# An attention, gating and expert kernel: value rows loaded straight from the input, and softmax denominators taken from a column of ones

## The reference

```python
for c in range(S // 32):
    k_full = concat(mem_k, k[:, :, max(0, 32*c - 16):min(S, 32*c + 40)])
    v_full = concat(mem_v, v[...same rows...])
    scores = q_c @ k_full.T / sqrt(64)
    a = exp(scores - scores.max(-1))
    a = a / (a.sum(-1) + 1e-9)
    out_c = a @ v_full
```

## Time and profile before

| | us |
|---|---|
| median of three runs | 2741.96 (2741.23 to 2748.13) |
| the profiled execution | 2741.23 |
| its span in the trace | 2739.5 |
| PE busy | 2662.7, 97% |
| DVE, ACT, POOL busy | 1388.3, 770.8, 516.0 |

### The profile page before, as it was taken

The page is one execution under the profiler, slowest core; times in us unless marked ns, Lnnn a source line. Parts: engine busy times, 40 slices in busy tenths (PEclk is TensorE's granted clock), DMA queues, the critical chain, the costliest instruction groups (busy, mean ns, idle before and its releaser), DMA issues.

```text
span 2739.5 us, 36851 instructions
## 1 busy us (share of the span) xinstructions
PE 2662.7 (97%) x15264; PEld 2196.0 (80%) x15264; DVE 1388.3 (51%) x2039; ACT 770.8 (28%) x1301; POOL 516.0 (19%) x440
## 2 busy tenths in 40 slices
PE   7779999999999999999999999999999999999999
PEld 6667878878777888888888888888888888888887
DVE  2454554454558454454564554544546544545544
ACT  3444332232333333333332221222222212222211
POOL 0036520020254545545430000000001000000000
PEclk8899999999999999999999999999999999999999
DMA  9946553433355565555545334333333443343342
GB/s 217 194 112 242 218 190 145 162 141 139 146 173 173 196 207 173 203 200 177 209 153 199 128 131 165 127 140 156 127 149 147 158 159 137 127 168 128 131 165 89
DMA packets 138454, 445.23 MB, mean 163 GB/s; under 512 B 34608, under 2 KB 94000, under 8 KB 106800
## 3 DMA queue, kind: packets, MB, share of 16 engines
q1 hardware_dynamic: 138288, 442.88, 45.9%
HBM read 315.97 MB, written 133.43 MB: 164 GB/s over the span
## 4 chain that ended last, share of the span: by engine, by line
PE 92%; DVE 3%; issue 2%; POOL 1%; ACT 1%; DMA 0%; DVEq 0%; ACTq 0%; POOLq 0%
PE bank L729 44%; PE bank L804 44%; PE bank L651 2%; PE bank L666 1%; PE bank L691 1%; PE bank L678 1%; POOL X L572 1%; DVE tmp L1232 1%; PE bank L701 0%; DVE Y L1265 0%; DVE Y L1323 0%; ACT X L987 0%; DVE hid L1328 0%; DVE hid L1384 0%; PE bank L706 0%
## 5 line engine op out<-in xcount | busy, mean ns | idle before, releaser
L729 PE MATMUL bank<-X,W 128*128 128x512 f32 x5550 | 1397.1, 390 | 14.8 <-ACT tmp L1035 4.9
L729 PEld LDWEIGHTS bank<-X,W 128*128 128x128 f32 x5550 | 1040.1, 188 | 240.4 <-issue 20.6
L804 PE MATMUL bank<-W,hid 128*128 128x512 f32 x4608 | 1153.7, 389 | 2.4 <-DVE Y L1262 2.4
L804 PEld LDWEIGHTS bank<-W,hid 128*128 128x128 f32 x4608 | 864.5, 188 | 182.3 <-DVE Y L1262 2.8
L1262 DVE SCALAR_TENSOR_TENSOR Y<-bank,gate,Y 128x512 f32<-128x512 f32 x720 | 539.7, 750 | 567.8 <-PE bank L804 560.4
L572 POOL TENSOR_TENSOR X<-Y,X 128x1024 fp32r<-128x1024 f32 x30 | 77.9, 2599 | 1025.1 <-ACT X L987 1025.0
L1093 ACT ACTIVATE hid<-tmp 128x512 fp32r<-128x512 f32 x192 | 121.3, 632 | 354.7 <-DVE tmp L1229 274.6
L804 PE MATMUL bank<-hid,W 128*128 128x512 f32 x864 | 219.5, 390 | 1.2 <-issue 1.2
L1031 ACT ACTIVATE tmp<-bank 128x512 f32<-128x512 f32 x132 | 78.8, 597 | 487.1 <-PE bank L729 487.1
L1384 DVE SCALAR_TENSOR_TENSOR hid<-bank,hid 128x512 fp32r<-128x512 f32 x192 | 132.7, 691 | 162.9 <-ACT hid L1093 162.8
L804 PEld LDWEIGHTS bank<-hid,W 128*128 128x128 f32 x864 | 162.4, 188 | 35.5 <-issue 1.6
(11 more groups left out here) (85 smaller groups left out, 1062.5 us busy)
## 6 DMA issues: line engine op xcount, KB each, us to landing
W<-w_kept SPq DMA_DIRECT2D x88, 1792.0 KB, 8.7
w_kept<-W SPq DMA_DIRECT2D x44, 1792.0 KB, 6.7
W<-w_kept SPq DMA_DIRECT2D x76, 1024.0 KB, 4.9
w_kept<-W SPq DMA_DIRECT2D x38, 1024.0 KB, 4.9
raw<-in_moe_w_dram SPq DMA_DIRECT2D x64, 512.0 KB, 6.4
Kr<-in_k_dram SPq DMA_DIRECT2D x12, 512.0 KB, 6.1
Qr<-in_q_dram SPq DMA_DIRECT2D x12, 512.0 KB, 7.8
Vw<-v_rows SPq DMA_DIRECT2D x48, 128.0 KB
```

The source lines that it names most:

```text
L729: last = nc.tensor.matmul(into[:, :], W1[:, c % 2, ws, w_slot, kc, :], X[:, pos, xs, kc, :], start=(start and kc == 0 and n == 0), stop=(k ...
L804: last = nc.tensor.matmul(into[:, :], lhsT, rhs, start=(j == 0 and n == 0), stop=(j == 1 and n == 2))
```

## The change

`v_rows`, `vm_rows` and the copies inside DRAM go. `load_v` reads `v` and `mem_v` directly, one chunk and one of its three kinds of rows at a time: 24 DMAs for a quad instead of six, each with rows of 64 elements (256 bytes) instead of 256 (1 KB). `Vw` has six slots instead of four, one for each quad of a batch, and each head gets a 65th column that POOL sets to one at the start. With it `weigh_v` yields the denominator as a 65th output column, DVE reads it from PSUM, and `denominators`, `esum` and `clear` go. The rows outside the sequence are never loaded; their values are cleared once at the start, and so are their ones. Two weight loads (`load_up(0)`, `load_up(1)`) move ahead of `load_v(5)`.

```diff
-            Vw = sb("Vw", [P, VS, 4, HP, HD], F32, first)
+            Vw = sb("Vw", [P, G, 4, HP, HD + 1], F32, first)
...
-            def rows_v(b, lo, hi, done):
-                for f in range(2):
-                    for s0, s1, at in ((lo, hi, lo), *([(0, LEFT, -LEFT)] if lo == 0 else []),
-                                       *([(S - RIGHT, S, S)] if hi == S else [])):
-                        sp.dma_start(v_rows[b, f, LEFT + at:LEFT + at + s1 - s0, :].rearrange("s (h d) -> s h d", h=HP),
-                                     v[b, f::2, s0:s1, :].rearrange("h s d -> s h d")).then_inc(done, 16)
...
             def load_v(r):
-                b, g, slot = r // G, r % G, r % VS
-                if r >= VS:
-                    sp.wait_ge(a_o, r - VS + 1)
...
-                for f in range(2):
-                    into = Vw[64 * f:64 * f + 64, slot].rearrange("p c h d -> p c (h d)")
-                    of = v_rows[b, f, g * QUAD:g * QUAD + QUAD, :].rearrange("(c s) n -> s c n", s=CHUNK)
-                    sp.dma_start(into[0:CHUNK], of).then_inc(s_v[slot], 16)
...
+                b, g = r // G, r % G
+                if b > 0:
+                    sp.wait_ge(a_o, r - G + 1)
+                for f in range(2):
+                    for c in range(4):
+                        start = g * QUAD + c * CHUNK - LEFT
+                        s0, s1 = max(start, 0), min(start + WIN, S)
+                        at = 64 * f + s0 - start
+                        sp.dma_start(Vw[at:64 * f + CHUNK, g, c, :, 0:HD],
+                                     v[b, f::2, s0:start + CHUNK, :].rearrange("h s d -> s h d")).then_inc(s_v[g], 16)
+                        at = 64 * f + BLK
+                        sp.dma_start(Vw[at:at + s1 - start - CHUNK, g, c, :, 0:HD],
+                                     v[b, f::2, start + CHUNK:s1, :].rearrange("h s d -> s h d")).then_inc(s_v[g], 16)
+                        at = 64 * f + CHUNK
+                        sp.dma_start(Vw[at:at + MEM, g, c, :, 0:HD],
+                                     mem_v[b, f::2].rearrange("h m d -> m h d")).then_inc(s_v[g], 16)
...
+            sp.wait_ge(s_zero, 8)
             load_v(0)
...
+            nc.gpsimd.memset(Vw[:, :, :, :, HD:HD + 1], 1.0).then_inc(s_zero, 1)
+            nc.gpsimd.memset(Vw[:, G - 1, 3, :, 0:HD], 0.0).then_inc(s_zero, 1)
+            pool.wait_ge(s_zero, 4)
+            for f in range(2):
+                nc.gpsimd.memset(Vw[64 * f:64 * f + LEFT, 0, 0], 0.0).then_inc(s_zero, 1)
+                ones = Vw[64 * f + 32:64 * f + 64, G - 1, 3, :, HD:HD + 1]
+                nc.gpsimd.affine_select(out=ones, in_=ones, compare_op=ALU.is_ge, fill=0.0, base=32 - RIGHT - 1,
+                                        pattern=[[0, HP], [0, 1]], channel_multiplier=-1).then_inc(s_zero, 1)
...
-            def clear(r):
-                pool.wait_ge(a_exp, r + 1)
...
             def weigh_v(r):
...
-                            last = nc.tensor.matmul(b_o[f][32 * c:32 * c + 32, hp * HD:(hp + 1) * HD],
+                            last = nc.tensor.matmul(b_o[f][32 * c:32 * c + 32, hp * (HD + 1):(hp + 1) * (HD + 1)],
                                                     PT[rows, hp, c * CHUNK:(c + 1) * CHUNK],
-                                                    Vw[rows, r % VS, c, hp, :], start=True, stop=True)
+                                                    Vw[rows, r % G, c, hp, :], start=True, stop=True)
...
-            def denominators(r):
-                dve.wait_ge(a_exp, r + 1)
...
             def quotients(r):
                 dve.wait_ge(a_o, r + 1)
+                for f in range(2):
+                    nc.vector.tensor_scalar(rsum[:, f, :], b_o[f][:, 0:HP * (HD + 1)].rearrange(
+                        "p (j n) -> p j n", j=HP)[:, :, HD], EPS, None, ALU.add).then_inc(a_den, 1)
+                dve.wait_ge(a_den, 2 * r + 2)
+                nc.vector.reciprocal(rsum[:, :, :], rsum[:, :, :]).then_inc(a_rs, 1)
                 dve.wait_ge(a_rs, r + 1)
```

More of the change, by code:

```diff
@@ L63, in build @@
     UNITS = 4 * TH + 1
-    VS = 4
     BLK = CHUNK + MEM
@@ L113, in build @@
             nmax = sb("nmax", [P, 2, HP], F32, first)
-            esum = sb("esum", [P, HP, 2], F32, first)
-            rsum = sb("rsum", [P, HP, 2], F32, first)
+            rsum = sb("rsum", [P, 2, HP], F32, first)
             KT1 = sb("KT1", [P, HP, KCOLS], F32, first)
@@ L131, in build @@
         w1_kept = nc.dram_tensor("w1_kept", [2 * V1 + V2, P, 4 * NP * P], F32).ap()
-        v_rows = nc.dram_tensor("v_rows", [B, 2, LEFT + S + 2 * RIGHT, HP * HD], F32).ap()
-        vm_rows = nc.dram_tensor("vm_rows", [B, 2, MEM, HP * HD], F32).ap()
         w2_kept = nc.dram_tensor("w2_kept", [V1 + V2, P, 4 * D], F32).ap()
@@ L148, in build @@
         s_q = [sem(f"s_q{i}") for i in range(TH)]
-        s_v = [sem(f"s_v{i}") for i in range(VS)]
-        s_vr = [sem(f"s_vr{i}") for i in range(TH + B - 1)]
+        s_v = [sem(f"s_v{i}") for i in range(G)]
         s_zero = sem("s_zero")
@@ L160, in build @@
         a_exp = sem("a_exp")
-        a_pad = sem("a_pad")
-        a_sum = sem("a_sum")
         a_pt = sem("a_pt")
@@ L293, in first_use @@
             return BUILDS.index(w) if w in BUILDS else None
[L297 to L301, removed]
         MK, KU, QU = range(3)
@@ L354, in load_mem, with load_v @@
                 sp.dma_start(Mk[:, :, :], mem_k[b].rearrange("h m d -> m h d")).then_inc(s_mk, 16)
-            def rows_v(b, lo, hi, done):
+            def load_v(r):
+                b, g = r // G, r % G
+                if b > 0:
+                    sp.wait_ge(a_o, r - G + 1)
                 for f in range(2):
-                    for s0, s1, at in ((lo, hi, lo), *([(0, LEFT, -LEFT)] if lo == 0 else []),
-                                       *([(S - RIGHT, S, S)] if hi == S else [])):
-                        sp.dma_start(v_rows[b, f, LEFT + at:LEFT + at + s1 - s0, :].rearrange("s (h d) -> s h d", h=HP),
-                                     v[b, f::2, s0:s1, :].rearrange("h s d -> s h d")).then_inc(done, 16)
-                    if lo == 0:
-                        sp.dma_start(vm_rows[b, f].rearrange("m (h d) -> m h d", h=HP),
-                                     mem_v[b, f::2].rearrange("h m d -> m h d")).then_inc(done, 16)
@@ L452, in _ @@
             load_q(0, 0)
-            rows_third(0)
             load_k(0, 1)
-            rows_third(1)
+            sp.wait_ge(s_zero, 8)
             load_v(0)
@@ L459, in _ @@
             load_v(1)
-            rows_third(2)
             load_q(0, 2)
@@ L466, in _ @@
             load_v(3)
-            rows_batch(1)
             load_k(1, 1)
@@ L470, in _ @@
             load_q(1, 1)
+            load_up(0)
+            load_up(1)
             load_v(5)
             load_k(1, 2)
-            load_up(0)
-            load_up(1)
             sp.wait_ge(s_wgz, 1)
@@ L487, in _ @@
                 if b < B and g == 3:
-                    rows_batch(b)
                     load_k(b, 1)
@@ L533, in _ @@
                                     base=0, pattern=[[-1, P]], channel_multiplier=1).then_inc(s_zero, 1)
+            nc.gpsimd.memset(Vw[:, :, :, :, HD:HD + 1], 1.0).then_inc(s_zero, 1)
[6 more added lines that the diff above has]
+                                        pattern=[[0, HP], [0, 1]], channel_multiplier=-1).then_inc(s_zero, 1)
+            pool.wait_ge(s_zero, 8)
             nc.gpsimd.memset(wg[:, :, :], 0.0).then_inc(s_wgz, 1)
@@ L536, in _ @@
             for c in range(KC):
-                pool.wait_ge(s_zero, 3 + c)
+                pool.wait_ge(s_zero, 9 + c)
                 done = nc.gpsimd.affine_select(out=fold[:, :], in_=fold[:, :], compare_op=ALU.not_equal, fill=1.0,
@@ L573, in operand_lo @@
                                         ALU.subtract).then_inc(x_lo, 1)
-            def clear(r):
-                pool.wait_ge(a_exp, r + 1)
[L578 to L591, removed]
             up_sums(0)
             up_lo(0)
[L594 to L599, removed]
+            for i in range(len(X_POOL)):
                 operand_lo(0, 0, i)
@@ L672, in transpose_p @@
                 pe.wait_ge(a_exp, r + 1)
-                if edge(r):
-                    pe.wait_ge(a_pad, edges_to(r))
                 if r > 0:
@@ L682, in weigh_v @@
                 pe.wait_ge(a_ptc, r + 1)
-                pe.wait_ge(s_v[r % VS], 6 * 16 * (r // VS + 1))
+                pe.wait_ge(s_v[r % G], 24 * 16 * (r // G + 1))
                 if r > 0:
@@ L822, in gates_fold @@
                 if t == 0:
-                    pe.wait_ge(s_zero, 3 + KC)
+                    pe.wait_ge(s_zero, 9 + KC)
                 for m in range(SUB):
@@ L1170, in quotients @@
                 for f in range(2):
-                    nc.vector.tensor_tensor(On[:, :, f, :],
-                                            b_o[f][:, 0:HP * HD].rearrange("p (j n) -> p j n", j=HP),
```

(5 more changed lines are left out.)

## The result

The changed kernel takes 2819.06 us (median of four runs, 2817.98 to 2820.31) against 2741.8, a ratio of 1.0276 with a 95% interval of 1.0259 to 1.0294. It is slower by 77 us. The forecast was 2812, within a range of 2788 to 2866.

A forecast was written before the change was run, and what follows sets the result against it. The attention stage, bound by transfers, would become bound by SP issuing 576 value DMAs: floor 241 plus 22 us puts the last at 263, a shift of 70.5; 2739.5 + 70.5 + 1.7 gives 2812 us, range 2788 to 2866.

The forecast's parts named there:

- The bound: Attention stage: bound by transfers before the change, by SP's issuing of DMAs after it, SP needing 241 us or more.
- T: Moment at which SP has issued the attention stage's last value DMA: 175 us before, forecast 263, between 241 and 316.
- SP's price of a DMA: SP's queue, value loads: time per DMA unchanged at a quarter of the size, 0.38 us each, 218.9 us for 576.
- The stops: SP's queue: pauses in issuing DMAs, taken as 22 us above the floor of 241 us.
- rival A: SP's queue: every value DMA costs 0.51 us, last one issued at 316, time 2865 us; chance 0.20.
- The DMA engines: Attention stage loads: 18 to 44 ns a packet, 123 to 203 us in all, below SP's 241, so not binding.
- Rival B: Attention stage: the busiest DMA engines bind instead of SP, at 44 ns a packet 263 us, time 2815; chance 0.17.
- What is late next: End of attention stage: last value matmuls run about 2.5 us after the last value DMA; everything behind shifts 70.5 us.
- T - 192.5: Shift of the last value matmuls and everything behind them, T + 2.5 - 195.0; 70.5 us at T = 263.
- Costed at nothing: DVE's reduction and POOL's selects, hidden in the attention stage, and the copies' leaving the DMA queue: worth nothing.
- C: Attention stage: faster, SP needing under 0.296 us from DMA to DMA, stage at PE's pace, time 2711; chance 0.03.
- D: Next stage: not moved by late values, as PE's first products need only the first eight quads; time 2742, chance 0.04.

The follow-up runs named there:

- e1: Changed kernel with the values' memory rows loaded once for three quads, by head: 448 value DMAs instead of 576, same 256-byte packets; 2782.8 us, 1.0152.
- e3: Kernel before with each value DMA cut in four: 576 value DMAs instead of 144, same 1 KB packets and copies inside DRAM; 2847.5 us, 1.0389.
- e7: Changed kernel with the odd heads' 288 value DMAs issued by POOL, the even heads' by SP; 2756.4 us, 1.0047.
- e4: Changed kernel with 96 tiny unused PE matmuls added ahead of each quad's value matmuls; 2861.7 us, 1.0441.
- e9: Changed kernel with 48 tiny unused PE matmuls added ahead of each quad's value matmuls; 2836.6 us, 1.0352.
- e5: Changed kernel with one value DMA taking one head over the chunks of two quads: 304 value DMAs, same 256-byte packets; 2742.6 us, 1.0000.
- e2: Changed kernel without the column of ones, denominators as in the kernel before; 2817.6 us, 1.0281.
- e6: Changed kernel with one value DMA taking one head over the chunks of three quads: 208 value DMAs; 2728.2 us, 0.9945.

## Why the prediction was right

**The bound.** The step from "the stage is bound by transfers" to "it will be bound by SP" held: T = 268.0 where 263 was forecast, and PE waits for values, not for keys. That the stage was bound by transfers before is read from a DMA share of 1.01 and 1.04; no run tested it by itself.

**SP's price of a DMA.** It was the term that carried the sum, 576 times 0.38 us = 218.9 us, and the new medians put it at 192 x (0.317 + 0.391 + 0.308) + 576 x 0.045 = 221. e1 and e3 change the number of DMAs and leave the packets, and T moves by 34 and 122 us. e7 leaves both and moves the issuing.

**The stops.** 22 us were taken between 0 and 75; they are 25.8 (the sum over 32 long issues of what is above 0.35 us). Right in size, but by luck: the 22 was a choice between two ends, and the reason was not in the text. The forecast saw the stops as something each DMA might cost and hoped for smaller packets. Three quarters of them come with instruction packets: e4 and e9 add these and get 22 and 14 more long issues, while e1 takes 128 DMAs away and gets no fewer. For that reason rival A (0.51 us for each DMA, T = 316) was wrong in kind: there is a stop every 8 us on average, however many DMAs stand between. The stop of the quad that A was read from, at 152.66, starts 0.1 us behind an instruction packet too.

**The DMA engines.** From 100 to 105 and from 200 to 205 us of the changed kernel nearly only value packets move (packets, MB, share):

```profile
q1 hardware_dynamic: 833, 0.19, 19.3%
```

```profile
q1 hardware_dynamic: 1232, 0.28, 24.9%
```

These are 19.3% x 80 / 833 = 18.5 and 24.9% x 80 / 1232 = 16.2 ns for a packet to SBUF, the few smaller ones that close a transfer counted in, at or below the low end of 18 to 44. Rival B needed 44 ns; it is out, and e5 confirms it.

**What is late next.** The landing took 1.4 us, not 2.5 (T to 269.41), and the first products were slower: the 12 matmuls behind the last values took 5.18 us, against 3.03 for the same 12 before. The stretches of the two, in the changed kernel and in the one before (columns as in the earlier trace rows):

```profile
270.50:275.70 5.20, 5.20 (x20) 4.08 (x15) 2.32 (x6) 0.00 (x0) 0.00 (x0) 0.55 1.00 396
```

```profile
195.80:198.80 3.00, 3.00 (x19) 2.44 (x15) 2.10 (x3) 0.00 (x0) 3.00 (x3) 1.00 0.02 5
```

The granted clock is 0.55 where it was 1.00: PE had waited for values up to then, and nearly all of those matmuls ran at the lower of its two levels, 1.2 instead of 2.4 GHz. Together 268.0 + 1.4 - 195.0 + 2.15 = 76.6, the shift that was seen. The formula T - 192.5 gives 75.5; that it comes so near is luck, as its two errors, -1.1 and +2.15, half cancel. Of the 7 us between forecast and time, 5 are T's, and 3.8 of these the stops.

**Costed at nothing.** The denominators, the ones, POOL's selects: e2 shows nothing within 3 us, as forecast. The copies inside DRAM: that they leave the DMA engines brought nothing, as forecast. That they leave SP's queue did: e3 keeps them, with as many value DMAs, and its T is 296.9 instead of 268.0. The forecast names SP's time for them and has the gain in its sum, where they have no term.

**C and D** did not occur. What is open: whether the earlier queries are all of the 14 us that e6 gains on e5. The wait of 10.9 us that goes would be most of it, but no kernel moved these loads alone at the end.

## What to carry to other kernels

Count DMA instructions before counting bytes. Here, where one engine issues them all, each costs about the same 0.3 to 0.4 us whether it moves 8 KB or 128 KB, and a stage may turn to being bound by issuing without any of its bytes changing, as in e3. The same packets can be grouped into DMAs in more than one way, so choose the grouping with the fewest instructions: the changed kernel took a chunk with all heads (24 a quad), while a head with all chunks (under nine a quad) loads the same packets and turned a loss of 2.8% into a gain of 0.5%. And measure a side idea alone: the column of ones, which took much of the edit, was worth nothing here.

## What the hardware showed that was not expected

- SP's DMA instructions stop for about 0.8 us beside most of the 16 KB instruction packets: up to T, 32 long issues with 32 packets in the changed kernel, 46 with 49 in e9, 54 with 63 in e4. SP, whose own instructions are the same in all three, was so slowed by 12 and 18 us by instructions added to PE.
- A packet of 256 bytes from DRAM to SBUF takes 16 to 18.5 ns of a DMA engine, about as much as inside DRAM (18 ns).
- POOL issues the same DMAs at 0.56 us each against SP's 0.35 to 0.44.
